# Attention in front of two expert layers: probabilities turned on VectorE, the weighted sum in row groups, k and q split before they are turned

## The reference

```
q_bucket = sum((q @ proj > 0) * 2**arange(6));  k_bucket the same from k
scores = where(q_bucket == k_bucket, q @ k.T / 8, -1e9)
attn = exp(scores - max) / (sum + 1e-9);  x = attn @ v
x: greedy choice of one of 8 experts per token (capacity 192 each), relu(x @ w1[e]) @ w2[e]
out = silu(x @ w_in) @ w_out
```

## Time and profile before

| | |
|---|---|
| median of 3 runs | 818.46 us (816.99 to 820.39) |
| the profiled execution | 819.84 us, its span 817.9 us |
| attention, to the last x product | about 294 us of the span |
| busy over the span | PE 97%, DVE 63%, ACT 33%, POOL 12% |
| granted TensorE clock, mean | 0.992 |

### The profile page before, as it was taken

How to read it: one execution, slowest core, us unless ns; L and a number is a source line. 1 busy time by engine, 2 the same in 40 slices (tenths; PEclk the granted TensorE clock), 3 DMA queues, 4 the chain that set the end, 5 groups by cost and what they waited for, 6 DMA issues and landing times.

```text
span 817.9 us, 14884 instructions
## 1 busy us (share of the span) xinstructions
PE 795.9 (97%) x5566; PEld 642.7 (79%) x5572; DVE 513.9 (63%) x1217; ACT 272.1 (33%) x586; POOL 100.1 (12%) x137
## 2 busy tenths in 40 slices
PE   8899999999999988999999999999999999999996
PEld 5667666666666645999999999998888788878885
DVE  6888888888888697888779773173332433243231
ACT  4566666666666621212212212221012111121101
POOL 4101221312123301011011100000000100010001
PEclk9999999999999989999999999999999999999999
DMA  5141624425141104344546338720000100010001
GB/s 117 40 102 21 139 58 86 96 45 131 44 107 55 36 21 168 138 173 136 201 130 206 136 129 300 262 103 0 1 1 5 46 0 0 0 51 0 0 0 52
DMA packets 73035, 68.27 MB, mean 83 GB/s; under 512 B 50752, under 2 KB 58944, under 8 KB 71968
## 3 DMA queue, kind: packets, MB, share of 16 engines
q1 hardware_dynamic: 69440, 60.43, 24.6%
q0 software_dynamic: 2208, 7.21, 2.7%
q10 hardware_dynamic: 1344, 0.04, 0.1%
HBM read 61.38 MB, written 6.29 MB: 83 GB/s over the span
## 4 chain that ended last, share of the span: by engine, by line
PE 91%; DVE 4%; issue 1%; DMA 1%; ACT 1%; POOL 1%; ACTq 0%; DVEq 0%; POOLq 0%
PE pt_ps L1501 16%; PE score_ps L1484 15%; PE pt_ps L1390 10%; PE pt_ps L1402 10%; PE pt_ps L1272 8%; PE pv_ps L1220 5%; PE score_ps L1208 4%; PE score_ps L1220 4%; PE score_ps L1209 4%; PE work_ps L1332 2%; PE score_ps L1181 1%; PE work_ps L1181 1%; DMA area<-x_rows,ids_now 1%; PE pt_ps L1229 1%; PE score_ps L1378 1%
## 5 line engine op out<-in xcount | busy, mean ns | idle before, releaser
L1501 PE MATMUL pt_ps<-y_s,w_in_s 128*128 128x512 f32 x576 | 137.8, 390 | 2.7 <-DVE y_s L1136 2.0
L1484 PE MATMUL score_ps<-w_out_s,gate_s 128*128 128x512 f32 x576 | 137.4, 389 | 0.0
L1501 PEld LDWEIGHTS pt_ps<-y_s,w_in_s 128*128 128x128 f32 x576 | 107.9, 188 | 26.1 <-DVE y_s L1136 2.8
L1484 PEld LDWEIGHTS score_ps<-w_out_s,gate_s 128*128 128x128 f32 x576 | 108.2, 188 | 22.4
L1154 DVE TENSOR_TENSOR gate<-pt_ps,sig 128x512 f32<-128x512 f32 x48 | 33.2, 692 | 146.3 <-ACT sig L648 146.3
L514 ACT ACTIVATE att_area<-att_area 128x768 f32<-128x768 f32 x96 | 90.0, 937 | 89.7 <-DVE att_area L852 89.7
L852 DVE TENSOR_SCALAR_CACHE_REDUCE att_area<-score_ps 128x768 f32<-128x768 f32 x96 | 91.8, 956 | 21.1 <-PE score_ps L1209 19.7
L1390 PE MATMUL pt_ps<-area,experts_w 128*128 128x192 f32 x512 | 97.6, 338 | 1.5 <-ACT area L608 1.2
L648 ACT ACTIVATE sig<-pt_ps 128x512 f32<-128x512 f32 x48 | 28.7, 598 | 210.5 <-PE pt_ps L1501 210.5
L1402 PE MATMUL pt_ps<-area,experts_w 128*128 128x192 f32 x512 | 87.2, 328 | 0.0
L1390 PEld LDWEIGHTS pt_ps<-area,experts_w 128*128 128x128 f32 x512 | 83.1, 192 | 2.1 <-ACT area L608 2.1
(11 more groups left out here) (208 smaller groups left out, 1025.2 us busy)
## 6 DMA issues: line engine op xcount, KB each, us to landing
experts_w<-in_moe_w SPq DMA_DIRECT2D x16, 2048.0 KB, 8.4
experts_w<-in_k SPq DMA_DIRECT2D x15, 384.0 KB, 4.4
experts_w<-in_q SPq DMA_DIRECT2D x15, 384.0 KB, 5.2
experts_w<-in_moe_w_in SPq DMA_DIRECT2D x8, 512.0 KB, 4.9
w_out_raw<-in_moe_w_out SPq DMA_DIRECT2D x4, 1024.0 KB, 8.1
att_area<-in_v SPq DMA_DIRECT2D x16, 192.0 KB, 2.4
x_rows<-att_area SPq DMA_DIRECT2D x8, 384.0 KB, 3.1
area<-x_rows,ids_now POOLq DMA_INDIRECT x16, 4.0
```

Source lines behind the costliest of these rows:

```text
L1484: done = nc.tensor.matmul(out_ps[m], gate_s[:, fo % RING_S, a, m * P:(m + 1) * P], w_out_s[:, fo, b, :], start=(fo == 0 and a + b == 0), s ...
L1501: done = nc.tensor.matmul(layer_ps[f % 2][:, 0:GT], w_in_s[:, a, w_cols], y_s[:, c, b, :], start=(c == 0 and a + b == 0), stop=(c == DC - ...
```

## The change

- **DVE turns the probabilities.** A DVE transpose turns blocks of 32x32 in place of the whole 128x128. One instruction per tile, 128x768, SBUF to SBUF. PE's transposes and the copies out of `pt_ps` are gone.
- **The weighted sum follows from it.** Keys now lie in four groups of 32 rows, so a product is 32 rows x 64 columns x 192, one of the four row groups (`a`) and one of the two column halves (`b % 2`), each row group to its own PSUM bank of `quad_ps`. 96 of them a head instead of 12. They stand at tiles 1, 2, 3 and 5, by `SHARE`. v is loaded four times, once per row group (`v_quarters`). ACT `turned` now gathers four banks, 768 columns. The x product is six matmuls of 72 columns instead of three of 144.
- **k and q are split before PE turns them.** POOL `split_rows` makes high and low parts in the natural layout, side by side, so one drain by ACT takes both. k's low part comes to lie in `k_parts` with the high one; `cross`, a DMA on SP, brings k's high part to the partitions of the bits' tile. Rows are loaded once, not doubled.
- **Bits.** ACT drains the raw products; POOL makes bits of both in `finish_bits`: one copy and three `tensor_scalar` of 64x768.
- Order: POOL does `finish_bits` of head h + 1, `split_rows` of head h + 2, the logits, and then the piece of `w_in`. In the opening `split_rows` of head 1 stands ahead of the first head's bits.

```
-    DE = 2 * (D + E)
+    DE = D + E
+    Q = 32
+    KB = S // Q
...
-    v_rows = v.rearrange("b h (p t) d -> (b h) p t d", t=T)
+    v_rows = v.rearrange("b h (m i t) d -> (b h) i m (t d)", t=T, i=Q)
...
+        quad_ps = ctx.enter_context(nc.psum_tensor("quad_ps", [P, 4 * 512], f32))
+        score_ps = [ctx.enter_context(nc.psum_tensor("score_ps", [P, 1024], f32)), quad_ps[:, 0:1024]]
+        pt_ps = [quad_ps[:, 1024:1536], quad_ps[:, 1536:2048]]
         pv_ps = ctx.enter_context(nc.psum_tensor("pv_ps", [P, 512], f32))
         work_ps = ctx.enter_context(nc.psum_tensor("work_ps", [P, 512], f32))
 
-        work_banks = [work_ps, score_ps[1][:, 0:512]]
-        pv_banks = [pv_ps, score_ps[1][:, 512:1024]]
...
+        QT = T * Q
+        sums_ps = quad_ps.rearrange("p (a n) -> p a n", a=P // Q)[:, :, 0:QT].rearrange("p a (t j) -> p a t j", t=T)
...
-                for rows, nat, loaded in ((k_rows, k_nat, s_k), (q_rows, q_nat, s_q)):
-                    src = rows[bass.ds(h, 1)].rearrange("a p t d -> p (a t) d")
-                    twice = src.unsqueeze(2).broadcast_to([P, T, 2, D])
-                    sp.dma_start(nat[p].rearrange("p t (r d) -> p t r d", r=2), twice).then_inc(loaded[p], 16)
+                sp.dma_start(k_nat[p][:, :, 0:D], head(k_rows, h)).then_inc(s_k[p], 16)
+                sp.dma_start(q_nat[p][:, :, D:P], head(q_rows, h)).then_inc(s_q[p], 16)
+
+            def cross(p, drained):
+
+                sp.wait_ge(s_work_free, drained)
+                sp.dma_start(k_bits[p][0:D, :].bitcast(f32), k_parts[p][D:P, :].bitcast(f32)).then_inc(s_cross[p], 16)
 
             def load_v(h, p):
-                sp.dma_start(v_nat[p], head(v_rows, h)).then_inc(s_v[p], 16)
+                src = v_rows[bass.ds(h, 1)].rearrange("a i m n -> i (a m) n")
+                for a in range(P // Q):
+                    sp.dma_start(v_quarters[p][Q * a:Q * (a + 1)], src).then_inc(s_v[p], 16)
...
+            load_qk(1, 1)
+            cross(0, 2)
             load_v(0, 0)
-            load_qk(1, 1)
             load_v(1, 1)
+            cross(1, PREP + 2)
...
+                act.wait_ge(s_work_full, w + 1)
+                if kind in ("k", "q"):
+                    dst, src = (k_parts if kind == "k" else q_parts)[p_next][:, cols], bank[:, 0:HALF]
+                else:
+                    dst, src = (k_bits if kind == "k_bits" else q_bits)[p_next][D:P, cols], bank[D:P, 0:HALF]
+                nc.scalar.activation(dst, src, ACT.Copy, scale=-SCALE if kind == "q" else 1.0).then_inc(s_work_free, 1)
...
-                nc.scalar.activation(weighted_t[p], pv_banks[p][:, 0:HALF], ACT.Copy).then_inc(s_turned, 1)
-
-            for i in range(PREP):
-                drain_work(PREP_KINDS[i], i % 2, i, i, 0, bank=first_banks[i % 4])
+                nc.scalar.activation(weighted_t.rearrange("p (t a j) -> p a t j", t=T, j=Q), sums_ps, ACT.Copy).then_inc(s_turned, 1)
...
-                        act.wait_ge(s_pt[1], n + 1)
-                        nc.scalar.activation(probs_t[p][t // TH][:, TH:T, t % TH, :],
-                                             pt_ps[1][:, 0:HALF].rearrange("p (a b) -> p a b", a=3), ACT.Copy).then_inc(s_ptc[1], 1)
...
+            def split_rows(h, p, loads):
+
+                for nat, loaded, raw, high, n in ((k_nat[p], s_k[p], slice(0, D), slice(D, P), 0), (q_nat[p], s_q[p], slice(D, P), slice(0, D), 1)):
+                    hold(loaded, 16 * loads + 16)
+                    nc.gpsimd.tensor_copy(nat[:, :, high].bitcast(f32r), nat[:, :, raw]).then_inc(s_split_step, 1)
+                    pool.wait_ge(s_split_step, 2 * (h - 1) + n + 1)
+                    nc.gpsimd.tensor_tensor(nat[:, :, raw], nat[:, :, raw], nat[:, :, high], ALU.subtract).then_inc(s_split, 1)
+                    hold(s_split, 2 * (h - 1) + n + 1)
...
+            def finish_bits(h, p, drained):
+
+                keep_high_of_q(p, drained)
+                hold(s_bit_step, 3 * h)
+                ks, qs = k_bits[p][D:P, :], q_bits[p][D:P, :]
+                hold(s_work_free, drained + 2)
+                nc.gpsimd.tensor_scalar(ks, ks.bitcast(f32), 0.0, -BIG, ALU.is_gt, ALU.mult).then_inc(s_bit_step, 1)
+                hold(s_bit_step, 3 * h + 1)
+                nc.gpsimd.tensor_scalar(ks, ks.bitcast(f32), k_shift[D:P, :], None, ALU.add).then_inc(s_bit_step, 1)
+                hold(s_bit_step, 3 * h + 2)
+                hold(s_work_free, drained + 4)
+                nc.gpsimd.tensor_scalar(qs, qs.bitcast(f32), 0.0, q_shift[D:P, :], ALU.is_lt, ALU.add).then_inc(s_bits, 1)
...
+            split_rows(1, 1, 0)
+            finish_first_bits()
...
+                        finish_bits(h + 1, 1 - p, PREP + 4 if first and p == 0 else preps_of(h + 1) + 2)
+                    if not last:
+                        split_rows(h + 2, p, g + 1)
...
-                        dve.wait_ge(s_pt[0], n + 1)
+                        dve.wait_ge(s_exp, n + 1)
                         if t == 0 and not first:
                             dve.wait_ge(s_pv, h - 1)
-                        nc.vector.tensor_copy(probs_t[p][t // TH][:, 0:TH, t % TH, :],
-                                              pt_ps[0][:, 0:HALF].rearrange("p (a b) -> p a b", a=3)).then_inc(s_ptc[0], 1)
-                        if t == 0 and not (first and p == 0) and not (last and p == 1):
-                            drain_work("k", 1, w - 1, high_of("k", 1, h + 1), 1 - p,
-                                       bank=bank_of(first, 1 - p, 9 if first else 8))
-                        elif (t - 1, 1) in ev:
-                            kind, half_, i, ahead = ev[(t - 1, 1)]
-                            drain_work(kind, half_, w, high_of(kind, half_, h + ahead), (p + ahead) % 2,
-                                       bank=bank_of(first, p, i))
+                        nc.vector.transpose(probs_t[p][:, t, :], probs[c % 3]).then_inc(s_pt, 1)
...
+            def weighted(h, p, b0, n, loads):
+
+                if n and b0 == 0:
+                    pe.wait_ge(s_pt, T * h + T)
+                    pe.wait_ge(s_v[p], 64 * loads + 64)
+                    pe.wait_ge(s_turned, h)
+                for b in range(b0, b0 + n):
+                    for a in range(P // Q):
+                        rows = slice(Q * a, Q * (a + 1))
+                        side = slice(D * (b % 2), D * (b % 2 + 1))
+                        done = nc.tensor.matmul(quad_ps[side, 512 * a:512 * a + QT],
+                                                v_quarters[p][rows, b % 4, D * (b // 4):D * (b // 4 + 1)],
+                                                probs_t[p][rows, :, Q * b:Q * (b + 1)], start=(b < 2), stop=(b >= KB - 2))
+                if n and b0 + n == KB:
                     done.then_inc(s_pv, 1)
...
+            SHARE = [0, 6, 6, 8, 0, 4]
...
-                        pe.wait_ge(s_exp, n + 1)
-                        for half in range(2):
-                            if not (first and c == 0):
-                                pe.wait_ge(s_ptc[half], n)
-                            for b in range(3):
-                                done = nc.tensor.transpose(pt_ps[half][:, b * P:(b + 1) * P],
-                                                           probs[c % 3][:, (3 * half + b) * P:(3 * half + b + 1) * P], ident[:, :])
-                            done.then_inc(s_pt[half], 1)
...
+                            weighted(h - 1, 1 - p, sum(SHARE[0:t]), SHARE[t], g if p else g - 1)
```

More of the change, by code:

```diff
@@ L746, in _, with pair @@
             split_proj()
-            finish_bits(0, 0, 0, 6)
+            split_rows(1, 1, 0)
+            finish_first_bits()
             more_constants()
-            def pair(g, first, last):
-                w = work_base(g)
+            def pair(g, first, last, beside=None):
                 for p in range(2):
@@ L754, in pair @@
                     ev = events(p, first, last)
-                    if (0, 0) in ev:
-                        finish_bits(h + 1, w, 1 - p, 6 if first and p == 0 else 4)
+                    if not (last and p == 1):
+                        finish_bits(h + 1, 1 - p, PREP + 4 if first and p == 0 else preps_of(h + 1) + 2)
+                    if not last:
+                        split_rows(h + 2, p, g + 1)
                     if last and p == 1:
@@ L761, in pair @@
                         add_logits(h - 2)
-                    w = w + len(ev)
+                    if beside is not None and p == 0:
+                        split_beside(beside, h)
             def split_beside(g, h):
@@ L950, in pair @@
                         dve.wait_ge(s_head_logits, h - 1)
[L951 removed]
+                        dve.wait_ge(s_x_free, h - 1)
                     if (5, 1) in ev:
@@ L1211, in scores @@
                 done.then_inc(s_scores, 1)
-            def weighted(h, p, b, loads):
-                if b == 0:
-                    for part in range(2):
-                        pe.wait_ge(s_ptc[part], T * h + T)
```

(8 more changed lines are left out.)

293 lines of the change are left out of this document (139 added, 154 removed).

## The result

| kernel | median | runs | ratio to before, 95% interval |
|---|---|---|---|
| before | 817.73 us | 816.55 to 820.39 | |
| changed | 896.53 us | 892.51 to 898.40 | 1.095, 1.091 to 1.100 |
| forecast | 790, range 776 to 827 | | |

A forecast was written before the change was run, and what follows sets the result against it. PE, busy 97%, was taken as the bound. Heads 0 to 4 give -9.1, ten more -21.6, opening +2: -28.7 on 819.84 makes 791.1; the median lies 1.4 below that execution, so 790, range 776 to 827.

The forecast's parts named there:

- the line on GpSimd: GpSimd's work per head, bit steps at 0.91 us each: 8.5 to 9.0 of 15.2 us, hidden.
- The clock: Attention: 1.2 GHz would void the sum; PE stays over nine tenths busy, so no case given.
- rival 2: GpSimd waits for DVE transposes on a shared path; bits about 1 us late at tile 4; 804 us, chance 0.09.
- Streaming of the weighted sum: PE's weighted matmuls, eight at a time: 4.3 us a head taken, between 3.89 and 4.80.
- Rivals 1, 4 and 5: Weighted sum: row groups overlap three-fold (802, chance 0.14); only four tiles in flight (833, 0.09); no overlap (above 920, 0.03).
- the rule of 3.07-fold overlap: Weighted sum on PE: the skill's 3.07x for four row tiles would make streaming 5.1 us.
- The tiles: Attention loop: each tile costs the larger of PE's and DVE's work, 2.05 to 2.74 us a tile.
- Rival 3: DVE transposes at half rate, 1.76 us each: DVE becomes the bound, 17.5 us a head, 825 us, chance 0.09.
- Head 15.2: Steady attention head: sum of its six tiles with streaming at 4.3, 15.2 us against 17.36 before.
- The lower bound: Attention head if PE alone sets it: 14.2 us a head, 776 us in all.
- PE's own sum: PE's work in one head: 7.74 + 4.3 + 1.24 = 13.3 us, no longer the whole answer.
- The opening's +2: Opening: GpSimd's bits for head 0 wait behind split_rows of head 1; first scores at 13.4, +2 us.

The follow-up runs named there:

- the filled run: Changed kernel with 22 matmuls on ones added before tile 4's scores in each head, GpSimd's slow forms kept: 863.63 us, ratio 1.056.
- the run with fast forms: Changed kernel with GpSimd's three bit operations of heads 1 to 15 as multiply-and-add, comparisons left out: 793.26 us, ratio 0.970.
- the best run here: Changed kernel with bits by Sign on ScalarE, four weighted blocks moved from tiles 1 and 2 to tile 5: 786.87 us, ratio 0.961.

## Why the prediction was wrong

**The step that failed** is the line on GpSimd: "one copy and three tensor_scalar of 64x768 at 0.91", with its conclusion "Little slack, nothing on the path". The row was a true measurement of the same size, type and engine, but of multiply-and-add; the change's operations are comparison-and-multiply, a lone addition, and comparison-and-add. They took 2.79, 2.21 and 2.86, so 7.9 us instead of 2.7. The term should have been given bounds like every other unseen operation, and its slack (0.4 us as it turned out) set against them. In steady heads the way from the start of k's first step to the end of q's is 8.43 us with the slow forms and 3.55 with the fast, where q's step also waited 0.6 for its drain: 4.9 more, less the slack 4.5 a head or 68 us in 15 heads, near the 70.4 of the filled run, which has the filling's own 3 to 6 in it.

**The clock**: "PE stays over nine tenths busy in the forecast, so I give that no case". True in the forecast, and void with the wait: 33 us more. A case with a wait on PE needs the clock's price added; no rival had it. The Trainium skill, "TensorE: Matmul & The Clock Gate", in the section "HAM oscillation — how this bites in real kernels", tells of a kernel whose PE waits for a DMA in each round and restarts each round at the lower clock. This trace agrees, with GpSimd in the DMA's place: 4.5 us of wait and a mean clock of 0.80 to 0.81 in each steady head.

**Right place, wrong cause**: what would show the forecast wrong was named, "scores of tile 4 released by GpSimd (rival 2)". That is what the trace shows, but not by rival 2's cause: no shared path of VectorE and GpSimd stretched these steps, 0.91 stayed 0.91 beside a transpose. Rival 2's price, 1 us a head, was far too low for the same place.

**The terms that hold**, read in the run with fast forms:
- Streaming of the weighted sum: 48 matmuls take 1.16 and 64 take 1.49 in the chain (both at full clock), so 16 more are 0.33, or 0.165 us for eight: all eight tiles run at once, 3.96 a head where 4.3 was taken and 3.89 was the lower bound. Rivals 1, 4 and 5 fall, the rule of 3.07-fold overlap among them. (The text's "about 0.35 us a group" fits eight of the source's matmuls, which are sixteen instructions; eight instructions start every 0.163.)
- The tiles, in the order of the maxima shown: forecast 2.74 (x drain), 2.35 (reciprocal), 2.05 (the bare loop), 2.71, 2.71, 2.32; measured 2.77, 2.18 (2.65 in every other head, for which the forecast had no term), 1.99, 2.75, 2.76, 2.39. Rival 3 falls with 0.974 for the transpose.
- Head 15.2 against 15.07; the whole 790 against 793.3 and 794.1. That this is so close is in part luck: streaming was taken 0.3 a head too long, the 2.65 was missing, and head 0 took 15.3 where 13.9 was taken. The lower bound has a slip as well: PE's own sum is given as 13.3 and then as 14.2, without the step between them; the best run here has heads of 14.4 and 14.7. The opening's +2 came as 2.1 to 2.5 (first maximum at 14.53 and 14.91, 12.42 before); in the changed kernel it is 14.72, with the first scores at 13.74 where 13.4 was forecast.

So the time of the changed kernel is that of the forecast's kernel, 793, plus some 70 for the late bits, plus some 33 for the clock.
